# One letter in a filter: which tasks stand between two score slots that share PSUM banks

## What is computed

```python
for t in range(S):
    kt, vt, rt, wt = (k[:, :, t], v[:, :, t], r[:, :, t], w[:, :, t])
    cur = np.einsum('bhd,bhe->bhde', u[None] * kt, vt)
    y[:, :, t] = np.einsum('bhd,bhde->bhe', rt, state + cur)
    state = wt[:, :, :, None] * state + np.einsum('bhd,bhe->bhde', kt, vt)
...
h = np.maximum(np.maximum(x @ w1, x @ w2), x @ w3)       # x: 3072 x 384, w1..w3: 384 x 768
x = (h @ w_out).astype(np.float32)                       # w_out: 768 x 384
...
h = x @ w_in                                             # w_in: 384 x 1024
e = np.exp(h - h_max)
sm = e / (np.sum(e, axis=-1, keepdims=True) + 1e-09)
solu = h * sm
ln = (solu - mu) / np.sqrt(var + 1e-06) * g_ln           # mu, var of solu along a row
return (ln @ w_out).astype(np.float32)                   # w_out: 1024 x 384
```

## Time and profile before

| | us |
|---|---|
| median of 3 runs | 764.0 |
| lowest and highest | 761.86 and 764.19 |
| the profiled execution, its time | 764.0 |
| its span, from the first to the last instruction | 761.9 |
| PE busy | 728.2 (96%) |
| DVE busy | 485.9 (64%) |
| ACT busy | 299.4 (39%) |
| POOL busy | 68.5 (9%) |
| mean granted clock of PE | 0.997 of full speed |

### The profile page before, as it was taken

One profiled execution on the slowest core, in us unless ns is written; L12 is line 12 of the kernel. 1 busy time (PEld: TensorE's weight loads), 2 busy tenths in 40 slices (PEclk: granted clock), 3 DMA queues, 4 the chain that ended last, 5 costly groups with the idle time before them and its releaser, 6 DMA issues.

```text
span 761.9 us, 22453 instructions
## 1 busy us (share of the span) xinstructions
PE 728.2 (96%) x9504; PEld 612.3 (80%) x9504; DVE 485.9 (64%) x942; ACT 299.4 (39%) x716; POOL 68.5 (9%) x180
## 2 busy tenths in 40 slices
PE   5899999999999999999999999999999999999987
PEld 4688999788888778888778888778888877888766
DVE  3788777895556786465788456679456578132480
ACT  3654543671332453322455313446133146111250
POOL 3131121100101101011101011001010000000000
PEclk9999999999999999999999999999999999999999
DMA  7563332355022156122045320134501004300043
GB/s 252 167 199 115 102 100 85 95 171 167 15 65 80 40 167 199 38 80 79 19 155 168 103 78 30 56 117 145 179 5 59 3 14 148 123 1 1 0 149 114
DMA packets 55107, 73.96 MB, mean 97 GB/s; under 512 B 7904, under 2 KB 41952, under 8 KB 55008
## 3 DMA queue, kind: packets, MB, share of 16 engines
q1 hardware_dynamic: 54448, 72.39, 29.9%
q10 hardware_dynamic: 560, 0.15, 0.1%
HBM read 48.32 MB, written 22.02 MB: 92 GB/s over the span
## 4 chain that ended last, share of the span: by engine, by line
PE 83%; DVE 5%; issue 3%; DMA 3%; ACT 2%; SPq 2%; POOL 0%; DVEq 0%; ACTq 0%; POOLq 0%
PE ps L716 17%; PE ps L786 15%; PE ps L718 15%; PE ps L717 15%; PE ps L625 12%; PE ps L711 3%; PE ps L701 2%; DMA zT<-z_turning 1%; PE ps L645 1%; DVE z_blocks L1011 1%; SPq L523 1%; DVE rk_sb L942 1%; DVE e_sb L1053 1%; DMA rk_sb<-in_rk 1%; DVE neg_max L1047 1%
## 5 line engine op out<-in xcount | busy, mean ns | idle before, releaser
L716 PE MATMUL ps<-xT,w_moe 128*128 128x512 f32 (+1 forms) x378 | 142.3, 376 | 1.0 <-issue 1.0
L786 PE MATMUL ps<-w_moe_out,zT 128*128 128x384 f32 x384 | 134.5, 504 | 8.6 <-ACT out_sb L921 5.0
L942 DVE TENSOR_TENSOR rk_sb<-rk_sb,decay 112x512 f32<-112x512 f32 x144 | 97.2, 693 | 64.4 <-PE ps L625 64.0
L717 PE MATMUL ps<-xT,w_moe 128*128 128x512 f32 (+1 forms) x378 | 136.7, 362 | 0.0
L718 PE MATMUL ps<-xT,w_moe 128*128 128x512 f32 (+1 forms) x378 | 136.6, 361 | 0.0
L786 PEld LDWEIGHTS ps<-w_moe_out,zT 128*128 128x128 f32 x384 | 118.7, 315 | 17.1 <-issue 6.8
L625 PEld LDWEIGHTS ps<-rk_sb 48*64 48x64 f32 x4224 | 84.1, 143 | 35.5 <-issue 28.4
L625 PE MATMUL ps<-rk_sb 48*64 48x32 f32 (+1 forms) x4224 | 96.3, 229 | 7.1 <-DVE rk_sb L942 5.1
L831 ACT COPY scoresT<-ps 16x128 f32<-16x128 f32 (+2 forms) x168 | 55.8, 332 | 106.0 <-PE ps L625 100.6
L716 PEld LDWEIGHTS ps<-xT,w_moe 128*128 128x128 f32 x378 | 72.0, 190 | 12.8 <-issue 1.1
L718 PEld LDWEIGHTS ps<-xT,w_moe 128*128 128x128 f32 x378 | 72.1, 191 | 11.0
(11 more groups left out here) (88 smaller groups left out, 992.4 us busy)
## 6 DMA issues: line engine op xcount, KB each, us to landing
rk_sb<-in_rk SPq DMA_DIRECT2D x24, 512.0 KB, 4.2
z_turning<-z_blocks SPq DMA_DIRECT2D x24, 512.0 KB, 3.0
zT<-z_turning SPq DMA_DIRECT2D x96, 128.0 KB, 2.9
w_sb<-in_w SPq DMA_DIRECT2D x24, 224.0 KB, 4.0
v_sb<-in_v SPq DMA_DIRECT2D x24, 192.0 KB, 4.2
k_turning<-k_blocks SPq DMA_DIRECT2D x18, 256.0 KB, 2.1
k_tok<-k_turning SPq DMA_DIRECT2D x72, 64.0 KB, 2.1
out<-out_sb SPq DMA_DIRECT2D x24, 192.0 KB, 2.6
```

What stands on the lines that cost most here:

```text
L716: nc.tensor.matmul(o, a[0], b[0], start=first, stop=False)
L717: nc.tensor.matmul(o, a[0], b[1], start=False, stop=False)
L786: last = nc.tensor.matmul(ps[:, OUT, 0:DM], zT[:, t % 2, :, c], w_moe2_out[:, c, :], start=(c == 0), stop=(c == J2 - 1))
L942: nc.vector.tensor_tensor(both, both, by, ALU.mult).then_inc(scaled, 1)
```

## The change

The filter of `bursts()` takes the letter t, DVE's turning of a z tile, besides those it had:

```diff
 def bursts():
 
     found, begun = [], False
-    for n, (kind, task) in enumerate(t for t in PROGRAM if t[0] in "sMudlo"):
+    for n, (kind, task) in enumerate(t for t in PROGRAM if t[0] in "sMudlto"):
         begun = begun or kind == "u"
         if kind == "s":
             if found and found[-1][0][-1][0] == n - 1 and len(found[-1][0]) < 2:
```

## The result

The changed kernel takes 773.44 us (median of 4 runs, 771.71 to 774.40), the kernel before beside it 764.1 (4 runs). The ratio is 1.0126, with a 95% interval of 1.0098 to 1.0152: slower by 9.3 us, where 6.5 were forecast, and 0.4 us beyond the upper end of the range. That 0.4 lies inside the interval of the measurement (which reaches down to 771.6), so the times alone don't say what was wrong; the traces do. The direction was right and so were both waits, to some hundredths of a microsecond. What failed is the term for the clock.

What follows compares the result with a forecast made beforehand. TensorE (PE), busy for 96% of the span, was taken to bound the kernel. Terms 3.51 + 2.38 - 0.86 + 1.5 = 6.5 us on 764.0 gave 770.5 us, range 767.5 to 773.0.

Steps and rivals of the forecast that it cites:

- the term for the clock: Products behind the new PE standstills: one fall to half rate, +1.5 us after the first, 0 after the second.
- What bounds the kernel, and the change part by part: PE, 96% busy, bounds; at about 158 to 176 us the split puts products that covered DVE's lag behind new waits.
- The two waits: PE idle 3.33 us before (7,6), 2.20 before (7,7), for DVE's masks of (8,1) and (8,2): +3.51 and +2.38 us.
- The swallowed DMA wait: Output product o1's wait for the DMA bringing zT disappears, as that transfer hangs on nothing that moved: -0.86 us.
- the cover for M's last scaling and for ACT's centring: Around o1: group 7's last scaling ends at 173.3, before M at 176.8; centring ends a microsecond before its transposition.
- the removed waits worth nothing: Waits on `masked` at (8,2), in M and at (8,3) were satisfied in time before, so removing them gains nothing.
- the sum: Without the clock, the place from (8,1) to M costs 3.51 + 2.38 - 0.86, which is +5.03 us.
- the exponential of tile 3: On ACT, behind the copy of (7,6): comes 0.7 us later, ends at 164.3, in time for DVE's read at 164.79.
- Whether the shift lasts: From 174 to 720 us: 0 comes back later, with all 5.0 us as the far bound.
- The second standstill: PE's 2.20 us wait before (7,7): no clock loss in the forecast, with 1.7 us kept in the range.
- a longer standstill: First wait, 3.33 us: low time begins 0.87 us earlier, saving 0.4 of it, so clock loss 1.3 to 1.7 us.
- Rival C: The clock falls at both new standstills: 770.5 + 1.7 = 772.2 us, chance 0.21.

Runs made afterwards that it cites:

- e10: The changed kernel unaltered, run again in more executions: 773.86 us (5 runs), ratio 1.0120 to the kernel before.
- e3: The changed kernel with dense, unused products on PE filling the two new standstills (14 behind slot (8,1), 9 behind (8,2)): 767.72 us, ratio 1.0052.
- e9: The changed kernel with both standstills filled by dense products, as in e3, run in more executions: 767.75 us (6 runs), ratio 1.0045.
- e6: The changed kernel with one more DVE instruction, result unused, ahead of the scaling and masks of slot (8,1): 774.33 us, ratio 1.0129.
- e2: The kernel before with only slots (8,2) and (7,7) parted, (8,1) and (7,6) staying one burst: 770.05 us, ratio 1.0077.
- e4: The changed kernel with the output product o0 moved ahead of the scores of slot (7,6) in the list: 771.82 us, ratio 1.0104.
- e1: The kernel before with only slots (8,1) and (7,6) parted, (8,2) and (7,7) staying one burst: 768.1 us, ratio 1.0054.
- e8: The kernel before with dense, unused products on PE at the start, ahead of early score bursts, and 10 near the end: 765.44 us (10 runs), ratio 1.0016.
- e7: The kernel before with one more DVE instruction, result unused, ahead of the scaling and masks of slot (8,1): 765.53 us (10 runs), ratio 1.0011.

## Why the prediction was wrong

**What bounds the kernel, and the change part by part**: right. The two waits were put at 3.33 and 2.20 us and measured 3.32 and 2.19 (3.31 and 2.19 in e10). The swallowed DMA wait, the cover for M's last scaling and for ACT's centring, and the removed waits worth nothing all came out; without falls of the clock the place costs 5.01 (e3, e9), where the sum had 5.03. One reading was off without harm: the exponential of tile 3 wasn't in time for DVE, which waited 0.21 us for it, and the 4.72 us that DVE then waited for PE cover that.

**Whether the shift lasts**: right. Nothing of it came back in the profile, where M to the last o is 0.74 us shorter, less than the 1.27 of the fall near the end that this execution was spared.

**The clock**: this is the step that failed. It took one fall for 1.5 us, the first, and 0 for the second; there were two, for 2.55 + 1.70 = 4.25, and 2.8 more is just what the median shows (9.3 against 6.5). Two things were wrong in it.

The second standstill was set to cost nothing because "the product ahead of it is dense". No row bore this out, and the row it was held beside spoke against it: the standstill of 2.46 ahead of the 7.25 has dense products of 128x512 right ahead of it too.

```profile
729.96 0.39 PE L718 MATMUL ps<-w_moe,h_x 128*128 128x512 f32 x1
```

What lies right ahead of the second standstill itself is the light scores of (8,2). In all three traces with a standstill of 2.19 us (changed kernel, e6, e10) the clock fell. The rule of the Trainium skill that was cited (TensorE: Matmul & The Clock Gate, section "HAM oscillation — how this bites in real kernels") comes from a kernel that waits about 3 to 5 us for its DMAs each time, and so it doesn't by itself say what 2.2 us do. Here the restart was paid at both standstills, with 2.55 and 1.70 us, and at the one near the end in some executions and not in others.

And a longer standstill was taken to save part of a low stretch of fixed length. It is the reverse. Where the clock fell while PE stood still, the low stretch was 6.8 us long (the first fall of the changed kernel and of e10, and those of e2 and e4), and where it fell after PE was back at work it was 3.4 (the second fall of the changed kernel and of e10, that of e1, the first of e6). So an earlier fall cost more. Rival C, 772.2, had the right count of falls; its 1.7 for the second was right, and its 1.5 for the first was a microsecond short.

**The rest of the margin.** The range ended 0.8 us above C, for a longer low clock. That was too little for a first fall of 2.55.

## What to carry to other kernels

Two tasks that share a buffer and one wait can be worth more than the wait they save. Here what stood behind the second one in the queue covered the reader, and when they were parted, that cover came after the wait. Ask of each new wait on a TensorE queue what independent product stands right behind it. And add to a new standstill of TensorE what the products behind it lose at half rate: here 5.0 us of waits became 9.2. How sure that loss is depends on the standstill. In the profiles of this study all six of 3.3 to 5.6 us and all three of 2.19 were followed by a fall; of those of 2.0 to 2.8 near the end, five of twelve were.

## What the runs showed of the hardware

The granted clock of a profile can miss a low stretch at its start. In the kernel before it is 1.00 up to 50 us, but the score rows of 32 took 1.08 us there and 0.67 later, and products of 128x256 ran at 0.41 and, from 52.47 on, at 0.28. In e8, where the clock had risen and fallen before, the same stretch is on record with 0.50. Durations of one form of product tell the clock more safely than the column. PE was busy for most of that stretch with scores and small products; the clock came up during the first products of 128x256, in the profiles of this study between about 50.1 and 56.1 us. That may be a part of the spread between executions; e2, where it came up at 56.1, is late at (8,1) (159.59), but e7 (160.11), where it was up by 52.7, is later still.

One open point: the two lengths of the low stretch, 3.4 and 6.8 us, went with whether the clock fell before or after PE resumed, but no run varied that by itself. One case is on the edge: in e6 the second fall is at 173.63, 0.02 us ahead of the start of (7,7), and its low stretch was 3.4 us long.
